# Sixteen steps with two pairs of G in every second one, and a shorter list of pieces for the first h chunk of batch 1

## What is computed

```python
    scores = scale * np.matmul(x, state.transpose(0, 1, 3, 2))
    ...
    a = np.exp(scores)
    a /= a.sum(-1, keepdims=True) + 1e-09
    xread = np.matmul(a, state)
    scores2 = scale * np.matmul(state, x.transpose(0, 1, 3, 2))
    ...
    sread = np.matmul(a2, x)
    return np.concatenate([xread, sread], axis=2).astype(np.float32)
...
    h = np.maximum(x @ w_in, 0.0)
    return (h * h @ w_out).astype(np.float32)
...
    a = x @ w1
    b = x @ w2
    h = a * b @ w3
    return (h @ w_out).astype(np.float32)
```

## Time and profile before

| | us |
|---|---|
| median of 3 runs (1244.4 to 1245.81) | 1245.15 |
| the profiled execution | 1243.96 |
| its span | 1242.3 |
| PE busy in it | 1229.1 |
| DVE, ACT busy | 813.9, 490.4 |
| start of the first pair of G | 7.89 |
| start of attention unit 15, the end of the sixteen steps | 76.49 |
| start of chunk 0 of batch 1 | 160.47 |

### The profile page before, as it was taken

How to read it: one execution, slowest core, us unless ns; L and a number is a source line. 1 busy time by engine, 2 the same in 40 slices (tenths; PEclk the granted TensorE clock), 3 DMA queues, 4 the chain that set the end, 5 groups by cost and what they waited for, 6 DMA issues and landing times.

```text
span 1242.3 us, 19672 instructions
## 1 busy us (share of the span) xinstructions
PE 1229.1 (99%) x7186; PEld 1078.5 (87%) x7186; DVE 813.9 (66%) x1447; ACT 490.4 (39%) x928; POOL 63.0 (5%) x109
## 2 busy tenths in 40 slices
PE   9999999999999999999999999999999999999998
PEld 6687878888888888888889999999999999999997
DVE  6877869676786966566544667575757565656541
ACT  6666656555555654454443422121212121212121
POOL 0001101011111100000000000000000000000000
PEclk9999999999999999999999999999999999999999
DMA  9977664443444432121214931010101010100220
GB/s 308 321 251 251 216 220 145 146 143 136 146 165 145 144 107 62 54 90 68 76 44 164 371 127 35 34 35 34 34 34 34 34 34 34 34 34 4 81 69 18
DMA packets 62836, 139.10 MB, mean 112 GB/s; under 512 B 5696, under 2 KB 6720, under 8 KB 62784
## 3 DMA queue, kind: packets, MB, share of 16 engines
q1 hardware_dynamic: 50176, 93.34, 22.3%
q0 software_dynamic: 12608, 45.10, 9.7%
HBM read 84.93 MB, written 53.48 MB: 111 GB/s over the span
## 4 chain that ended last, share of the span: by engine, by line
PE 96%; DVE 1%; DMA 1%; issue 0%; ACT 0%; SPq 0%; POOL 0%; DVEq 0%; ACTq 0%; POOLq 0%
PE ps_y L681 47%; PE ps_h L681 28%; PE ps_t L681 19%; DMA raw<-in_w_T 1%; PE ps_h L742 1%; PE ps_t L705 1%; PE ps_y L742 0%; DVE t L1313 0%; DVE v_lo L1223 0%; PE ps_t L742 0%; ACT v_hi L968 0%; SPq L503 0%; DVE X_lo L1223 0%; ACT t L968 0%; DVE stage L1331 0%
## 5 line engine op out<-in xcount | busy, mean ns | idle before, releaser
L968 ACT CAST v_hi<-t 128x512 fp32r<-128x512 f32 (+1 forms) x216 | 129.1, 598 | 443.9 <-DVE t L1223 443.0
L1223 DVE TENSOR_TENSOR v_lo<-t,v_hi 128x512 fp32r<-128x512 f32 (+1 forms) x216 | 143.1, 662 | 118.9 <-ACT v_hi L968 112.1
L681 PE MATMUL ps_y<-v_hi,X_hi 128*128 128x512 f32 (+1 forms) x576 | 218.9, 380 | 0.3 <-DVE v_lo L1223 0.3
L681 PE MATMUL ps_y<-v_lo,X_hi 128*128 128x512 f32 (+1 forms) x576 | 217.5, 378 | 0.0
L681 PE MATMUL ps_y<-v_hi,X_lo 128*128 128x512 f32 (+1 forms) x576 | 217.5, 378 | 0.0
L1223 DVE TENSOR_TENSOR t<-t 128x256 f32<-128x256 f32 (+1 forms) x272 | 143.5, 547 | 98.9 <-ACT t L1066 96.1
L1066 ACT ACTIVATE t<-ps_h 128x512 f32<-128x512 f32 (+1 forms) x144 | 82.5, 573 | 151.9 <-PE ps_h L681 151.4
L681 PEld LDWEIGHTS ps_y<-v_hi,X_lo 128*128 128x128 f32 x576 | 108.4, 188 | 20.3
L681 PEld LDWEIGHTS ps_y<-v_hi,X_hi 128*128 128x128 f32 x576 | 108.5, 188 | 20.1 <-issue 0.7
L681 PEld LDWEIGHTS ps_y<-v_lo,X_hi 128*128 128x128 f32 x576 | 108.5, 188 | 19.2
L1223 DVE TENSOR_TENSOR t<-t,ps_t 128x256 f32<-128x256 f32 (+1 forms) x132 | 72.6, 550 | 47.3 <-PE ps_t L681 33.5
(11 more groups left out here) (225 smaller groups left out, 2793.0 us busy)
## 6 DMA issues: line engine op xcount, KB each, us to landing
raw<-g_scratch SPq DMA_DIRECT2D x64, 256.0 KB
raw<-in_moe_w_in SPq DMA_DIRECT2D x32, 256.0 KB
raw<-in_x_T SPq DMA_DIRECT2D x32, 256.0 KB
raw<-in_x_tok SPq DMA_DIRECT2D x32, 256.0 KB
y_scratch<-stage POOLq DMA_DIRECT2D x8, 1024.0 KB, 6.3
s_scratch<-top POOLq DMA_DIRECT2D x32, 256.0 KB, 2.6
s_scratch<-E_lo POOLq DMA_DIRECT2D x32, 256.0 KB, 3.4
raw<-y_scratch SPq DMA_DIRECT2D x8, 1024.0 KB, 5.4
```

Source lines behind the costliest of these rows:

```text
L681: mm = nc.tensor.matmul(dst, w, m, start=first and n == 0, stop=last and n == 2)
L968: return nc.scalar.copy(dst, src)
L1223: return nc.vector.tensor_tensor(dst, a, b, op)
```

## The change

**Pairs.** `pairs_in(k)` says which pairs step k has: one in steps 0 and 1, two (k and k + 1) in the even steps from 2 on, none in the odd ones. The w_in pieces move with them, so an even step's list of pieces has two. In the steps 5, 7, 9, 11 and 13 what `beside` holds now comes ahead of the w3 unit. Attention units 3 and 4 are now both in step 5, 12 and 13 both in step 13, and the xT pieces come one step earlier.

**Banks.** In the steps even pairs use `ps_h` and odd ones `ps_t`; each waits for the pair two before it. So pairs and attention units share `ps_t`, and waits are added between them: attention unit 3 for the drain of pair 5, unit 12 for that of pair 13, unit 15 for that of pair 15, pair 7 for the copies of units 3 and 4, and pair 15 for those of 12 and 13.

**Batch 1.** `g_ready` at f = 0 waits only up to the piece ("G", 1, 1), the second of the batch's G, and for all of them at f = 2. For the later batches the same code has no other effect than to ask for less at f = 0.

```diff
+        def pairs_in(k):
+
+            return [k] if k < 2 else [k, k + 1] if k % 2 == 0 else []
+
         def step_pieces(k):
 
-            return ([("piece", "w_in", k)] + ([("piece", "wout2", k)] if k < KG else []) + [("piece", "w3T", k)])
-
-        beside = {1: [("att", 0)], 3: [("piece", "xT", 0, 0), ("piece", "xT", 1, 0)],
...
+            return ([("piece", "w_in", p) for p in pairs_in(k)] + ([("piece", "wout2", k)] if k < KG else [])
+                    + [("piece", "w3T", k)])
+
+        beside = {1: [("att", 0)], 2: [("piece", "xT", 0, 0), ("piece", "xT", 1, 0)],
...
-            order += [("pair", k), ("wp", k)] + beside.get(k, [])
+            if k in (5, 7, 9, 11, 13):
+                order += beside[k] + [("wp", k)]
+            else:
+                order += [("pair", p) for p in pairs_in(k)] + [("wp", k)] + beside.get(k, [])
...
-            return ps_h[:] if p < STEPS else (ps_h[:], ps_y[:, 0:2], ps_y[:, 2:4], ps_t[:])[p % 4]
+            return (ps_h, ps_t)[p % 2][:] if p < STEPS else (ps_h[:], ps_y[:, 0:2], ps_y[:, 2:4], ps_t[:])[p % 4]
 
         def last_in_banks(p):
 
-            return p - 1 if p <= STEPS else p - 4 if p >= STEPS + 4 else -1
+            if p < STEPS:
+                return p - 2
+            return {STEPS: STEPS - 2, STEPS + 1: -1, STEPS + 2: -1, STEPS + 3: STEPS - 1}.get(p, p - 4)
...
+                if p == 7:
+                    pe.wait_ge(att_free[0], uses(0, 0))
+                    pe.wait_ge(att_free[1], uses(0, 1))
+                if p == STEPS - 1:
+                    pe.wait_ge(att_free[0], uses(0, 2))
+                    pe.wait_ge(att_free[1], uses(0, 3))
...
                 if what[0] == "att":
+                    if what[1] == 3:
+                        wait_drained(pe, 5)
                     if what[1] == 12:
                         pe.wait_ge(ident_ready, 1)
+                        wait_drained(pe, 13)
+                    if what[1] == 15:
+                        wait_drained(pe, 15)
...
+                ahead = tile0_slots if r0 == R_1 and isinstance(i, int) else tile_slots
+                behind = flat(ahead)[flat(ahead).index(("G", 1, 1)) + 1:]
+
                 def ready(f):
                     if f == 0:
+                        pe.wait_ge(piece_split, i * 2 * PT + r0 - len(behind))
+                    if f == 2:
                         pe.wait_ge(piece_split, i * 2 * PT + r0)
```

More of the change, by code:

```diff
@@ L296, in build_program @@
         STEPS = N_PAIRS // BG
+        def pairs_in(k):
+            return [k] if k < 2 else [k, k + 1] if k % 2 == 0 else []
         def step_pieces(k):
-            return ([("piece", "w_in", k)] + ([("piece", "wout2", k)] if k < KG else []) + [("piece", "w3T", k)])
-        beside = {1: [("att", 0)], 3: [("piece", "xT", 0, 0), ("piece", "xT", 1, 0)],
[L303 to L306, removed]
+            return ([("piece", "w_in", p) for p in pairs_in(k)] + ([("piece", "wout2", k)] if k < KG else [])
+                    + [("piece", "w3T", k)])
+        beside = {1: [("att", 0)], 2: [("piece", "xT", 0, 0), ("piece", "xT", 1, 0)],
+                  3: [("piece", "xT", 2, 0), ("piece", "xT", 3, 0)], 5: [("att", 3), ("att", 4)], 6: [("att", 5)],
+                  7: [("att", 6)], 8: [("att", 7), ("piece", "x", 0, 0)], 9: [("att", 8), ("piece", "x", 1, 0)],
+                  10: [("att", 9), ("piece", "x", 2, 0)], 11: [("att", 10), ("piece", "x", 3, 0)], 12: [("att", 11)],
+                  13: [("att", 12), ("att", 13), ("piece", "G", 0, 0)], 14: [("piece", "G", 1, 0)],
                   15: [("piece", "G", 2, 0), ("piece", "G", 3, 0)]}
```

## The result

| | before | after |
|---|---|---|
| median, us (14 runs each, on the same chip) | 1244.49 | 1247.55 |
| lowest and highest | 1243.1, 1246.31 | 1244.0, 1249.23 |
| ratio to before, 95% interval | | 1.0022 [1.0013, 1.0031] |
| the profiled execution | 1243.96 | 1248.58 |
| its span | 1242.3 | 1247.0 |

The change makes the kernel slower by 0.2%. The page of after: engine table, and the chain that ended last (rows 1 of before).

A forecast was written before the change was run, and what follows sets the result against it. The prediction took PE's own instructions plus its idle time to bound the kernel. Its terms, -2.9 - 2.4 + 4.4 + 0.0 = -0.9 us, gave a median of 1244.2, with a range of 1241.0 to 1247.0.

The forecast's parts named there:

- The clock: Whole kernel: PE's granted clock was 1.00, the 2.4 GHz level, in every stretch looked at, so it was given no term.
- The rest of the sixteen steps: After the stall at attention unit 3: DVE drains pair 13 by 63.6, before unit 12 needs its bank; costed at 0.
- the cover of 1.0 us: Attention unit 12: DVE drains pair 13 1.0 us before PE needs the bank; each us beyond that costs one.
- my signs of being wrong: w3T 5 lands before 29 or after 31.5; pair 13 drained after PE reaches unit 12; PE's batch-1 lead lasts.
- The stall at unit 3: Attention unit 3: PE waits from 28.46 to 32.87 for DVE's drain of pair 5 behind w3T 5, +4.4 us.
- Rival 1: Transfers before unit 3 run without the two slow DMA stretches: stall 1.9, sum -3.4, time 1241.8; chance 30%.
- Visits: Sixteen steps: nine visits to G instead of sixteen, each losing 0.41 us, so -2.9 us.
- Pair waits: Sixteen steps: drain and piece waits of 3.2 us go, 0.5 and 0.3 come back, net -2.4 us.
- my walk: PE's forecast timeline through the sixteen steps, with 15.3 us from pair 12 to unit 15, which starts at 75.5.
- Batch 1: First h chunk starts 1.9 us earlier, but the wait returns at the first y chunk: 0.0, between 0 and -1.9.
- Rival 2: Batch 1: drains of ps_y come earlier because ACT and DVE did wait for PE; -2.8, 1242.4; chance 6%.
- Rival 3: Attention unit 3: w3T 5 lands later, a loss above 0.2% from 33.6 on; +2.7, 1247.9; chance 7%.

The follow-up runs named there:

- the kernels with the filler: Fourteen zero-product matmuls ahead of attention unit 3's wait: on the changed kernel 1245.75 us, 1.0015; on it without the batch 1 part 1245.70 us, 1.0014.
- The drain-first kernel: Changed kernel with pairs 4 and 5 listed ahead of step 5's pieces, so DVE drains pair 5 before waiting for w3T 5: 1242.06 us, 0.9985.
- the kernel with split visits: Changed kernel with pairs 4 and 5 ahead of step 5's pieces, plus pair k + 1 behind w3 unit k in steps 6, 8, 10: single run, 1244.92 us.
- the first four experiments: Changed steps alone 1247.54 us; batch 1 part alone 1243.86; changed kernel with pairs 4, 5 ahead of step 5's pieces 1242.06; with zero-product matmuls before unit 3 1245.75.

## Why the prediction was wrong

- **The clock (the step that failed).** "PE's granted clock is 1.00 ..., so the clock is no term here" was read from a kernel whose longest wait is 1.75 us, and carried over to one into which my own sum put a stall of 4.4. It costs 2.55 us in the profiled run, and the kernels with the filler are 1.7 and 1.8 us faster by the median than those without it that ran beside them. With that term alone the forecast would have been 1246.0.
- **The rest of the sixteen steps, costed at 0, failed too: +2.0.** I let DVE walk from pair 7 to pair 13 as one block of 23.5 us with no wait of its own, and had it done by 63.6. But DVE stood idle for w_in 13, which came late (2.26 us in the row above), and had the transposes of aT, an x piece and w3T 13 between it and the drain of pair 13. "If the cover of 1.0 us is gone (a late piece of w_in)" named the mishap, and "DVE drains pair 13 later than PE comes to unit 12", one of my signs of being wrong, came true; the price belonged in the sum. Why the total is the same when w_in 13 is in time is not shown. The terms as the runs have them, -0.9 + 1.8 + 2.0 + 0.4 (pair 21) = +3.3, come near the 3.1 between the medians.
- **The stall at unit 3: right.** Mechanism, place (28.1 against 28.46) and size (3.48 and 4.36 against 4.4) are as forecast, and w3T 5 is cast between 29 and 31.5. Rival 1, the clean transfers at 30%, came in part in the first profile: w3T 5 is cast at 29.22, 1.0 us sooner than forecast, and where before has 247 and 179 GB/s in its two slow stretches, after has one milder one, 273 and 287 GB/s from 16 to 20 us. The wait is a term with a spread of about a us from execution to execution.
- **Visits: right.** Nine of them, 0.43 us each against 0.41. **Pair waits:** PE waits for drains of pairs only once, 0.23 us at pair 3, up to step 11. The drain-first kernel, which has neither the stall nor the low clock, bears both terms out together: from its first pair to unit 15 it takes 65.88 us against 68.60 before, -2.7. Without the 2.2 by which its last steps are longer than my walk (17.51 us against 15.3) and one wait of 0.5 at w3 unit 7 that is -5.5, against -5.3 in the sum.
- **Batch 1: right to 0.1 us** (1.64 us instead of 1.75, h chunk 3 unmoved), and its 0.0 with it. Rival 2 was rightly put low: the chain on ACT and DVE doesn't wait for PE. What I did not say is that its order was open to an edit, and that this was the gain to be had.
- **Rival 3**, the slower case, had the right place and the wrong mechanism. It needed w3T 5 to land after 33.6; it was cast at 29.2 and at 30.9, and the time was lost behind the wait.

What stays open: why loads come at other times in another execution of the same kernel (w3T 5 is cast at 29.22 in one profile of the changed kernel and at 30.86 in the other; pair 13 waits 0.68 us for w_in 13 in the first and not at all in the second), and when exactly a short wait costs the clock (below).

## What to carry to other kernels

A new stall of PE of several us has two prices: its length, and the matmuls behind it at the 1.2 GHz level. Count both before a wait is added, and look at the granted clock of every stretch that follows a wait, since the waits view won't show it. When work is moved in a list that several engines follow, walk the queue of the issuing engine as well: here a load that two stores went ahead of came later, and that cost more than the two waits that were taken away. And when a wait only moves to the next consumer, look at where that consumer's releaser stands in its queue; moving four copies made 1.9 us of gain out of an edit worth nothing.

## What the runs showed of the hardware that I had not expected

Waits of nearly the same length do and don't cost the clock. Behind 3.48, 3.52 and 4.36 us of idle the granted clock was 0.50 each time. Of twelve waits between 1.43 and 2.00 us that I looked at in the profiles of ten kernels, two had it fall to 0.50 (1.81 in after; 1.56 in the kernel with split visits, where a second wait of 0.24 us follows) and ten, the longest of 2.00 us, kept 1.00. Here is the one of 2.00 (the kernel with the filler) with its stretch, and a stretch behind the one of 1.56:

```profile
171.45 0.50 PE L691 MATMUL ps_y<-v_hi,X_hi 128*128 128x512 f32 x1 [2.00 <-ACT stage L998]
```

```profile
171.00:173.00 2.00, 1.55 (x6) 1.09 (x7) 2.00 (x4) 2.00 (x5) 0.00 (x0) 1.00 0.71 191
```

```profile
45.00:46.00 1.00, 1.00 (x3) 0.31 (x1) 1.00 (x2) 0.85 (x2) 0.00 (x0) 0.50 1.01 315
```

The low clock also goes with the spread of the runs: the changed kernel's lie from 1244.0 us at a mean granted clock of 1.000 to 1248.6 and 1248.8 at 0.995. An estimate from these numbers: while PE is busy at half speed, the time lost is (1 - clock) x time. Over its fourteen runs the mean clock is 0.9971, against 0.9991 for before (over the 30 runs beside the first four experiments), which gives 3.6 against 1.1 us, 2.5 of the 3.1 us between the two medians. It is an upper bound. The clock is given to three digits, and a part of the low time falls on PE's idle time: for the profiled execution the estimate gives 6.2 us, where the two stretches above lost 2.55 + 1.7.
